# First four attention steps in another order, three casts moved to ScalarE, buffers of their own for chunk 1, a low part moved behind a normalisation

## What is computed

```python
# attention: batch 4, 8 heads, 576 positions, head size 64, window 64
scores = scale * q @ k.T;  masked to 0 <= i - j < 64;  attn = softmax(scores);  x = attn @ v
# block A (d_ff 1536)
xn = x / rms(x) * rms_g
x = (silu(xn @ w_gate) * (xn @ w_val)) @ w_out
# block B (d_ff 2048)
h = x @ w_in
out = (h * sigmoid(1.702 * h)) @ w_out2
```

## Time and profile before

| | |
|---|---|
| median of 3 runs | 904.75 us (903.81 to 905.58) |
| the profiled execution | 904.1 us, its span 901.6 us |
| TensorE matmul busy | 889.1 us, 99% |
| VectorE busy | 539.6 us, 60% |
| ScalarE busy | 398.5 us, 44% |
| GpSimd busy | 82.2 us, 9% |
| granted TensorE clock, mean | 0.998 |

### The profile page before, as it was taken

One profiled execution on the slowest core, in us unless ns is written; L12 is line 12 of the kernel. 1 busy time (PEld: TensorE's weight loads), 2 busy tenths in 40 slices (PEclk: granted clock), 3 DMA queues, 4 the chain that ended last, 5 costly groups with the idle time before them and its releaser, 6 DMA issues.

```text
span 901.6 us, 14706 instructions
## 1 busy us (share of the span) xinstructions
PE 889.1 (99%) x5372; PEld 771.3 (86%) x5372; DVE 539.6 (60%) x1256; ACT 398.5 (44%) x941; POOL 82.2 (9%) x114
## 2 busy tenths in 40 slices
PE   8899999999999999999999999999999999999998
PEld 7799888888888888888888899999999999999997
DVE  6886634334333343433336578887788788867663
ACT  5676333343333423334123354545464554545442
POOL 6234001030010300113000000000000000000000
PEclk9999999999999999999999999999999999999999
DMA  7672111102111021100500222121432122241201
GB/s 253 205 218 96 51 51 51 50 24 74 51 50 51 24 73 51 51 25 1 186 1 24 94 96 69 60 81 47 164 117 94 48 74 67 67 145 47 71 24 70
DMA packets 41078, 69.75 MB, mean 77 GB/s; under 512 B 3632, under 2 KB 13872, under 8 KB 41008
## 3 DMA queue, kind: packets, MB, share of 16 engines
q1 hardware_dynamic: 39600, 67.12, 23.0%
q10 hardware_dynamic: 1408, 1.70, 0.6%
HBM read 59.38 MB, written 9.44 MB: 76 GB/s over the span
## 4 chain that ended last, share of the span: by engine, by line
PE 94%; DVE 3%; ACT 2%; issue 1%; POOL 1%; POOLq 0%; ACTq 0%; DVEq 0%
PE ps L631 16%; PE ps L633 15%; PE ps L632 15%; PE ps L825 7%; PE ps L826 7%; PE ps L824 7%; PE ps L767 7%; PE ps L763 7%; PE ps L765 6%; PE ps L612 2%; PE ps L584 2%; PE ps L598 2%; DVE w_all L1197 1%; ACT prob L867 0%; DVE sig L1235 0%
## 5 line engine op out<-in xcount | busy, mean ns | idle before, releaser
L631 PE MATMUL ps<-x_hi,w_all 128*128 128x512 f32 (+1 forms) x480 | 179.4, 374 | 0.2 <-DVE x_lo L1137 0.2
L633 PE MATMUL ps<-x_lo,w_all 128*128 128x512 f32 (+1 forms) x480 | 176.7, 368 | 0.0
L632 PE MATMUL ps<-x_hi,w_all 128*128 128x512 f32 (+1 forms) x480 | 176.7, 368 | 0.0
L826 PE MATMUL ps<-w2out,hB 128*128 128x512 f32 x288 | 113.0, 392 | 0.0
L825 PE MATMUL ps<-w2out,hB 128*128 128x512 f32 x288 | 112.9, 392 | 0.0
L824 PE MATMUL ps<-w2out,hB 128*128 128x512 f32 x288 | 112.0, 389 | 0.0
L631 PEld LDWEIGHTS ps<-x_hi,w_all 128*128 128x128 f32 x480 | 90.4, 188 | 18.4 <-issue 3.0
L633 PEld LDWEIGHTS ps<-x_lo,w_all 128*128 128x128 f32 x480 | 90.4, 188 | 15.3
L632 PEld LDWEIGHTS ps<-x_hi,w_all 128*128 128x128 f32 x480 | 90.4, 188 | 14.6
L1235 DVE SCALAR_TENSOR_TENSOR sig<-sig,ps 128x512 f32<-128x512 f32 x48 | 32.9, 686 | 107.1 <-ACT sig L981 107.1
L631 PE MATMUL ps<-h_hi,w_all 128*128 128x512 f32 (+1 forms) x240 | 90.4, 376 | 1.8 <-DVE hid L1244 1.6
(11 more groups left out here) (144 smaller groups left out, 1557.0 us busy)
## 6 DMA issues: line engine op xcount, KB each, us to landing
wstage<-in_w_b SPq DMA_DIRECT2D x48, 512.0 KB, 3.7
wstage<-in_w_a SPq DMA_DIRECT2D x36, 256.0 KB, 3.2
vwin<-in_v_win SPq DMA_DIRECT2D x32, 256.0 KB, 3.9
kwin<-in_k_t SPq DMA_DIRECT2D x32, 160.0 KB, 3.3
x2raw<-x_scratch SPq DMA_DIRECT2D x3, 1536.0 KB, 7.5
out_dram<-yB SPq DMA_DIRECT2D x18, 256.0 KB, 4.4
qtok<-in_q_t SPq DMA_DIRECT2D x34, 128.0 KB, 2.6
x_scratch<-wstage SPq DMA_DIRECT2D x3, 1024.0 KB, 4.2
```

The source lines that it names most:

```text
L631: pe.matmul(out_, w[:, 0, cols], xh, start=first, stop=False, **flags)
L632: pe.matmul(out_, w[:, 1, cols], xh, start=False, stop=False, **flags)
L633: return pe.matmul(out_, w[:, 0, cols], xl, start=False, stop=last, **flags)
L826: ins = pe.matmul(y, hB_of(g, chunk, 1)[:, rows], w[:, 0, chunk, :], start=False, stop=last)
```

## The change

It has four parts.

- The first steps. TensorE transposes step 2 before it multiplies step 1, transposes step 3 before it multiplies 2, and does the four parts of chunk 0 in one piece behind the product of step 3; two pairs of the small matmuls go. ScalarE makes the four squares together behind the last `x_hi`. The semaphore of the copied transposes is split in two, one for VectorE's copies and one for ScalarE's.
- Casts. (0,1), (1,1) and (2,1) go from GpSimd to ScalarE. The order of the low parts of the first three chunks changes to `FIRST_SPLITS`; SyncE's and TensorE's waits follow it through `splitsA`.
- Buffers. Chunk 1's scaled gate lies in the second half of `ss`, its tanh and silu in `sq`. Both scaled gates are made together, then both tanhs.
- In tile 0 at c = 2 the low part of (4,0) stands behind the normalisation of step 5 and not before silu.

```diff
@@ places @@
+        def scaled_of(c):
+            return ss[:, GT:2 * GT] if c == 1 else gsc
+        def silu_of(t, c):
+            return sq[:, :] if (t, c) == (0, 1) else sig[:, 0:TILES_A[t][1]]
@@ counts @@
+        FIRST_SPLITS = ((0, 0), (0, 1), (1, 0), (1, 1), (2, 0), (0, 2), (2, 1), (1, 2), (2, 2))
         def splitsA(c, m):
-            return 3 * c + m + 1
+            return FIRST_SPLITS.index((c, m)) + 1 if c < 3 else 3 * c + m + 1
+        CASTS_BY_ACT = ((0, 1), (1, 1), (2, 0), (2, 1)) + tuple((c, m) for c in range(3, CA) for m in range(2))
+        CASTS_BY_POOL = ((0, 0), (1, 0), (0, 2), (1, 2)) + tuple((c, 2) for c in range(2, CA))
@@ GpSimd @@
             normalise(2)
-            weights_hi_A(0, 1)
             normalise(3)
-            weights_hi_A(0, 2)
             weights_hi_A(1, 0)
             add_early_square(1)
-            weights_hi_A(1, 1)
-            weights_hi_A(1, 2)
+            weights_hi_A(0, 2)
             add_early_square(2)
             add_early_square(3)
-            weights_hi_A(2, 1)
+            weights_hi_A(1, 2)
             weights_hi_A(2, 2)
@@ TensorE @@
             keep_busy(3, 2)
+            transpose_probs(2)
             probs_by_v(1)
-            transpose_probs(2)
+            transpose_probs(3)
             pe.wait_ge(max_ready, EARLY)
-            keep_busy(4, 2)
             probs_by_v(2)
-            transpose_probs(3)
-            first_chunk_part(0)
             probs_by_v(3)
-            for d in range(1, DC):
+            for d in range(DC):
                 first_chunk_part(d)
@@ ScalarE @@
             first_x_hi(0)
+            weights_hi_by_act(0, 1)
+            copy_probT(2)
             first_x_hi(1)
-            copy_probT(2)
-            first_square(0)
             copy_probT(3)
-            first_square(1)
             first_x_hi(2)
-            first_square(2)
             first_x_hi(3)
+            for s in range(EARLY):
+                first_square(s)
+            weights_hi_by_act(1, 1)
             nc.scalar.preload_act_table_set(LN_SET)
-            first_square(3)
             weights_hi_by_act(2, 0)
             act.wait_ge(consts_ready, 1)
             inverse_rms(0)
+            weights_hi_by_act(2, 1)
...
-                wait(act, hidA_made, n)
+                wait(act, hidA_made, n if (t, c) != (0, 1) else 0)
...
-                    tanh_A(t, c)
+                    if (t, c) != (0, 1):
+                        tanh_A(t, c)
+                    if (t, c) == (0, 0):
+                        tanh_A(0, 1)
@@ VectorE @@
             weights_lo_A(0, 0)
+            reciprocal_of_sum(3)
             evacuate_probT(1)
-            reciprocal_of_sum(3)
             dve.wait_ge(g_loaded, 16)
             first_x_lo(0)
             weights_lo_A(0, 1)
             first_x_lo(1)
-            weights_lo_A(0, 2)
+            weights_lo_A(1, 0)
             first_x_lo(2)
-            weights_lo_A(1, 0)
             first_x_lo(3)
             weights_lo_A(1, 1)
+            weights_lo_A(2, 0)
+            weights_lo_A(0, 2)
+            weights_lo_A(2, 1)
             weights_lo_A(1, 2)
-            weights_lo_A(2, 0)
-            weights_lo_A(2, 1)
...
-                    if t == 0:
+                    if t == 0 and c != 1:
                         scale_gate(c)
+                    if t == 0 and c == 0:
+                        scale_gate(1)
...
-                    if split is not None and c > 0:
+                    if split is not None and c > 0 and c != 2:
                         weights_lo_A(split, 0)
...
+                    if split is not None and c == 2:
+                        weights_lo_A(split, 0)
                     if split is not None and c > 0:
                         weights_lo_A(split, 1)
```

More of the change, by code:

```diff
@@ L204, in fused_attention_mlps @@
         probs_transposed = sem("probs_transposed")
+        first_probT_ready = sem("first_probT_ready")
         probT_ready = sem("probT_ready")
@@ L255, in wait, with wait_probT @@
                 eng.wait_ge(s, value)
+        def wait_probT(eng, n):
+            if n <= 2:
+                wait(eng, first_probT_ready, n)
+            else:
+                eng.wait_ge(probT_ready, n - 2)
         def slotA(c):
@@ L261, in raw @@
             return wstage[:, (3 * u + m) * DM:(3 * u + m + 1) * DM]
+        FIRST_SPLITS = ((0, 0), (0, 1), (1, 0), (1, 1), (2, 0), (0, 2), (2, 1), (1, 2), (2, 2))
         def splitsA(c, m):
-            return 3 * c + m + 1
+            return FIRST_SPLITS.index((c, m)) + 1 if c < 3 else 3 * c + m + 1
+        CASTS_BY_ACT = ((0, 1), (1, 1), (2, 0), (2, 1)) + tuple((c, m) for c in range(3, CA) for m in range(2))
+        CASTS_BY_POOL = ((0, 0), (1, 0), (0, 2), (1, 2)) + tuple((c, 2) for c in range(2, CA))
         def cast_by_act(c, m):
-            return (c, m) == (2, 0) or (c > 2 and m < 2)
+            return (c, m) in CASTS_BY_ACT
         def casts_so_far(by_act, c, m):
-            return sum(cast_by_act(*at_) == by_act for at_ in itertools.product(range(CA), range(3)) if at_ <= (c, m))
+            return (CASTS_BY_ACT if by_act else CASTS_BY_POOL).index((c, m)) + 1
         A11, A12, A22, S1, S2, S3, S4 = range(COMBOS)
@@ L576, in scores @@
                 elif s % 2 == 0:
-                    pe.wait_ge(probT_ready, s)
+                    wait_probT(pe, s)
                     pe.wait_ge(ln_done, home_of(s)[0])
@@ L591, in transpose_probs @@
                 if s < EARLY:
-                    wait(pe, probT_ready, s - 1)
+                    wait_probT(pe, s - 1)
                 else:
@@ L606, in probs_by_v @@
                 pe.wait_ge(v_loaded[slot(s)], 16 * uses(s))
-                pe.wait_ge(probT_ready, s + 1)
+                wait_probT(pe, s + 1)
                 for m in range(GB // 2):
@@ L620, in sum_squares @@
                     pe.wait_ge(early_sums, EARLY - 1)
-                    pe.wait_ge(probT_ready, EARLY - 1)
+                    wait_probT(pe, EARLY - 1)
                     pe.matmul(ps[:, ATT_BANK, 0:n], ones[:, :], ss[:, 0:n], start=True,
@@ L662, in gate @@
                     pe.wait_ge(x_lo_ready, 2)
-                    pe.wait_ge(probT_ready, EARLY)
+                    wait_probT(pe, EARLY)
                 elif t == 0 and c == 2:
@@ L1132, in evacuate_probT @@
                 dve.wait_ge(probs_transposed, s + 1)
-                nc.vector.tensor_copy(probT_of(s), pt_of(s)).then_inc(probT_ready, 1)
+                nc.vector.tensor_copy(probT_of(s), pt_of(s)).then_inc(first_probT_ready, 1)
             def first_x_lo(s):
@@ L1234, in silu_A @@
                 dve.wait_ge(sigA_ready, n + 1)
-                nc.vector.scalar_tensor_tensor(out=sig[:, 0:w], in0=sig[:, 0:w], scalar=1.0,
-                                               in1=gsc[:, :] if t == 0 else gate_of(t, c),
+                nc.vector.scalar_tensor_tensor(out=silu_of(t, c), in0=silu_of(t, c), scalar=1.0,
+                                               in1=scaled_of(c) if t == 0 else gate_of(t, c),
                                                op0=ALU.add, op1=ALU.mult).then_inc(siluA_done, 1)
@@ L1243, in hidden_A @@
                 wait(dve, hidA_lo, n)
[L1244 removed]
+                nc.vector.tensor_tensor(hid[:, 0:w], val_of(t, c), silu_of(t, c),
                                         ALU.mult).then_inc(hidA_made, 1)
```

5 lines of the change are left out of this document (2 added, 3 removed).

## The result

The changed kernel takes 908.13 us (median of 6 runs, 907.73 to 908.93); beside it the kernel before took 904.40 us (6 runs). The ratio is 1.0042, with a 95% interval of 1.0030 to 1.0054: slower by 3.7 us. The forecast was 905.0, 0.25 above the kernel before, and its range ended at 907.0.

A forecast was written before the change was run, and what follows sets the result against it. TensorE was taken as the bound, busy 889.1 of 901.6 us. The profiled 904.1, plus 0.2 at the scores of step 6 and 0.65 from profiled run to median, gave 905.0 us; range 902.2 to 907.0.

The forecast's parts named there:

- SyncE's queue: Loads behind (2,2) go out late, from about 21.8; (3,0) lands 0 to 0.3 us late for VectorE, 0.1 added.
- rival (a): Load of (3,0) takes 6 us, its cast comes 2.7 us after VectorE wants it: 907.1 us; chance 0.12.
- The scaled gate: VectorE's first scaled gate, behind ScalarE's cast of (2,1) and two low parts, at 25.8 (25.5 to 26.4); before, 23.86.
- the chain to `hidden_A`: On VectorE and ScalarE, chunk 1's `hidden_A` starts 4.25 us after the first scaled gate; before, 5.27.
- The stall of TensorE: TensorE waits for k before the scores of step 4, about 3.5 us, costing nothing at first.
- the gain of the first steps: Reordered first four steps bring the sum of squares 1.27 us earlier; spent before the scaled gate, behind the table load.
- this table load has no drain: ScalarE's table load before the cast of (2,1) costs 1.28 us without a drain; a drain would add 1.4 us.
- the moved low part: Low part behind step 5's normalisation: its transposes stay at 37.6 to 37.7, scores of step 6 at 42.2 to 42.4.
- The sum of squares: On TensorE after the first four steps, at 20.6 instead of 21.87, a gain of 1.27 us.
- (b): TensorE's clock falls where TensorE is the bound, near 41.6, putting 1.7 us on the path: 906.7 us; chance 0.12.
- (c): Aim met: scaled gates by 23.6 or earlier, projection waits for nothing; 898.8 us, or 901.9 for half; chance 0.16.
- The low clock: Clock falling in TensorE's stall before the scores of step 4: TensorE ends at 32.5, not 30.8, covered by later waits.

The follow-up runs named there:

- e16_third_held_9: Changed kernel with q, k, v of steps 4 and 5 loaded ahead of (2,2) and the load of (3,0) held until the ninth split: 909.07 us.
- e2_weights_first: Changed kernel with only the loads of (3,0) and (3,1) issued ahead of that of (2,2): 905.56 us.
- e1_loads_first: Changed kernel with q, k, v of steps 4 and 5 and the loads of (3,0) and (3,1) ahead of that of (2,2): 905.16 us.
- e6_loads_and_cast: Changed kernel with q, k, v of steps 4 and 5, (3,0) and (3,1) loaded ahead of (2,2), and ScalarE's cast of (2,1) ahead of the table load: 902.73 us.
- e4_clock_kept: Changed kernel with 14 small matmuls on ones filling TensorE's stall before the scores of step 4: 906.77 us.
- e8_before_low_part: Kernel before with only the low part of (4,0) moved behind the normalisation of step 5: 903.70 us.
- e11_e6_no_low_part: e6_loads_and_cast with the low part of (4,0) put back ahead of silu 2: 902.85 us.
- e15_third_held_8: Changed kernel with q, k, v of steps 4 and 5 loaded ahead of (2,2) and the load of (3,0) held until the eighth split: 905.59 us.

## Why the prediction was wrong

**The step that failed** is the one on SyncE's queue: "Part (3,0) lands at 28.3 if it takes 3.3 ... 0 to 0.3 us late. I add 0.1". The mechanism was named and its term mis-sized: VectorE waited 2.34 us for (3,0), not 0.1. Two numbers in it were off. The queue was released at 22.66, not at 21.8, so (3,0) went out at 25.88, not 25.0. The 21.8 had no walk behind it. The sixth split stands behind the fifth, (2,0), which waited for ScalarE's cast, and that cast stands behind the first table load. ScalarE, then VectorE with both splits:

```profile
18.74 1.28 ACT L982 ACT_TABLE_LOAD   x1
20.04 0.62 ACT L919 CAST w_all<-wstage 128x512 fp32r<-128x512 f32 x1
```

```profile
20.69 1.94 DVE L1214 TENSOR_TENSOR w_all<-wstage,w_all 128x512 fp32r<-128x512 f32 x2 [1.10 <-ACT w_all L919]
```

And the load took 5.1 us, not 3.3, a figure for which no row was given. This was rival (a), with a chance of 0.12, and the argument against it ("nothing is in flight when SyncE starts again") was the mistake: in these traces what counts is what is issued just ahead of a load, and that was seven others. The table of loads of the changed kernel, from 22.6 to 31 us (KB each, median us from issue to landing):

```profile
wstage<-in_w_a SPq DMA_DIRECT2D x7, 256.0 KB, 5.3
vwin<-in_v_win SPq DMA_DIRECT2D x2, 256.0 KB, 4.8
kwin<-in_k_t SPq DMA_DIRECT2D x2, 160.0 KB, 3.7
```

The kernel before has the same row in the same place, 19.7 to 24 us, and in it the load of (3,0) itself (19.78, the tile `wstage` from 19.7 to 19.8). The step should have rested on them, and not on the 3.3 us:

```profile
wstage<-in_w_a SPq DMA_DIRECT2D x5, 256.0 KB, 6.0
...
DMA to landing us min/median/max: 6.2/6.2/6.2
```

That these 6.2 us made nobody wait is why no list of waits shows them: its cast starts only at 26.59, when ScalarE comes to it. And the first of that row, (2,2) at 16.56, landed after 2.7 us there too, so an idle queue at the start does not help the eighth load. A load with nothing in flight ahead of it took 2.7 us also in e16_third_held_9 (29.90 to 32.60 above), although five more were issued behind it before it landed. By the Trainium skill (DMA: Bandwidth & Descriptors, Anatomy of one DMA), a transfer takes some 2.0 us and its bytes at 436 GB/s, a fit for loads that GpSimd issues; for 256 KB that is an estimate of 2.6 us. The first load of a row agrees; for the eighth the formula gives half of what was measured, and the windows above show 332 GB/s and a DMA share of 0.96 from 26 to 33. The eight loads from (2,2) to (3,0) bring 2 x 256, 2 x 128, 2 x 160 and 2 x 256 KB, 1.6 MB; at those 332 GB/s that is an estimate of 4.9 us of moving.

**The sum, term by term.** The prediction had chunk 1's `hidden_A` 0.9 us later (1.0 with the 0.1), and it was 3.56. The scaled gate gave +0.2 (26.01 for 25.8), the chain to `hidden_A` +0.1 (6.68 less the wait of 2.34 is 4.34, for 4.25), the wait 2.34. The 3.56 became 2.96 at the transposes of step 5, where I had 0 to 0.1 left of my 1.0, and 2.97 at the scores of step 6: 0.6 of it was covered.

**What was right.** Rival (a)'s mechanism and its mark (VectorE's wait for (3,0) from 29.29). It had (3,0) landed at 31.0 and cast at 31.7 (30.98 and 31.60) and VectorE's shift at 0.9 + 2.7 = 3.6 (3.56). Its landing time met the measured one partly by luck, since it issued the load 0.9 us too early and gave it 6 us for 5.1. Its time of 907.1 was 1.0 us too low, because it let the chain cover 1.3 of the shift, and the traces show 0.6, and because of the second loss below. The stall of TensorE (3.92 us for "about 3.5") and that it costs little by itself: e2_weights_first has it in full and is 0.4 us from e1_loads_first. That the gain of the first steps is spent before the scaled gate, by the cast behind the table load: e6_loads_and_cast against e1_loads_first prices it at 2.4 us. That this table load has no drain: the cast stands 0.01 us behind it (24.15). That the moved low part gives nothing. The sum of squares was half right, at 21.12 for 20.6: a gain of 0.75 us and not 1.27. Rivals (b) and (c) did not come: the granted clock is 1.00 from 38 to 43, and the first scaled gate was later than 23.6.

**The low clock** was put down as covered. It came (0.51 from 26 to 33) and made the projection late, 33.87 for the 33.33 of e4_clock_kept, the run that puts its worth at 0.3 to 1.4 us. That part of the step stands on weaker ground than I gave it, but it did not decide.

**A second loss** of 0.6 us, between the scores of steps 6 and 8 (12.77 us apart; 12.16 before), was not in the prediction. VectorE after the change, the first normalisation of step 6, a low part, silu and `hidden_A`, and under it GpSimd:

```profile
49.52 1.03 DVE L1146 TENSOR_TENSOR prob<-prob,rrec 128x512 f32<-128x512 f32 x1
50.47 1.23 DVE L1214 TENSOR_TENSOR w_all<-wstage,w_all 128x512 fp32r<-128x512 f32 x1
51.62 0.83 DVE L1252 SCALAR_TENSOR_TENSOR sig<-sig 128x256 f32<-128x256 f32 x1
52.48 0.42 DVE L1261 TENSOR_TENSOR hid<-ps,sig 128x256 f32<-128x256 f32 x1
```

```profile
50.08 1.07 POOL L536 TENSOR_TENSOR ss<-ss,sq 128x256 f32<-128x256 f32 x1
51.10 1.07 POOL L545 CAST w_all<-wstage 128x512 fp32r<-128x512 f32 x1
```

From the normalisation to `hidden_A` it is 2.96 us; the kernel before needs 2.43 (46.46 to 48.89), with its silu at 0.41 us and GpSimd's cast (46.90 to 47.97) over before silu starts at 48.44. In the changed kernel the cast runs beside silu. All eighteen traces part the same way: silu takes 0.41 us in the seven where that cast has ended, and 0.82 to 0.83 in the eleven where it still runs. The moved low part brings it about in both pairs that differ by it alone (0.41 before and 0.82 in e8_before_low_part; 0.41 in e11_e6_no_low_part and 0.82 in e6_loads_and_cast), though not always: in e4_clock_kept it is moved too, and silu takes 0.41. No run moves GpSimd's cast by itself, so which engine hinders which is argued and not shown.

## What to carry to other kernels

Where a change alters the order in which something is completed, go through every queue that waits on a count of it, and list what stands behind that wait: here a wait on SyncE, an engine that computes nothing, cost more than all else that the change did. Read a load's landing time from the same load behind the same loads, not from the fastest row, since a queue that has been held lets everything go at once; and read it from issue to landing, since a load that is slow and not waited for stands in no list of waits. And when a part of a change seems worth nothing, look at what waits behind it: the earlier cast gave nothing that the time could tell with the load late and 2.4 us without, and the first steps gave nothing without the casts.

## What the runs showed of the hardware

- A load of 256 KB landed 2.7 us after its issue with nothing in flight ahead of it ((2,2) of the changed kernel; (3,0) in e15_third_held_8 and e16_third_held_9, with further loads issued right behind it), and 5.1 us after it with seven others issued in the 3.2 us before it ((3,0) of the changed kernel).
- A hold of (3,0) by count that sent it out about 0.7 us later than the changed kernel does cost nothing (e15_third_held_8). With nothing in flight ahead of it, the later issue landed earlier, 30.43 (29.2 without the late start) against 30.98.
- TensorE's granted clock fell to about 0.5 in the changed kernel in a stall of 3.92 us (1.00 from 20 to 26, 0.51 from 26 to 33), and did not fall in the same place when small matmuls filled the stall (e4_clock_kept: 1.00). In e16_third_held_9 TensorE stood from 27.5 until its projection at 34.89; the clock was at 0.96 from 27 to 30 us and at 0.50 from 30 to 38.
- The `silu` of 128x256 that VectorE makes beside step 6 took 0.41 us in the seven traces where GpSimd's cast had ended before it, and 0.82 to 0.83 us in the eleven where the cast ran beside it.
